# First routing of a retention + MoE + GLU kernel: counts of 32 bins by one product per tile of tokens, the digit by a product with ones

## The reference, cut to what matters

```python
logits = x @ w_gate                       # 3072 x 8
order = np.argsort(-logits.flatten())
for idx in order:                         # best pair first
    tok, e = idx // E, idx % E
    if assigned[tok] >= 0 or counts[e] >= cap: continue
    assigned[tok] = e; counts[e] += 1
h = np.maximum(x[mask] @ w1[e], 0.0); out[mask] = h @ w2[e]      # for each expert
y = (1 / (1 + np.exp(-(out @ w_gate2)))) * (out @ w_val) @ w_out
```

## Time and profile before

| | |
|---|---|
| median of 3 runs | 1074.85 us (1074.79 to 1075.24) |
| profiled execution, its own time | 1075.28 us |
| its span | 1073.5 us |
| PE busy | 1029.4 us (96%) |
| DVE busy | 704.0 us (66%) |
| ACT busy | 326.2 us (30%) |
| POOL busy | 122.6 us (11%) |
| moved by DMA | 107.69 MB |

### The profile page before, as it was taken

The page is one execution under the profiler, slowest core; times in us unless marked ns, Lnnn a source line. Parts: engine busy times, 40 slices in busy tenths (PEclk is TensorE's granted clock), DMA queues, the critical chain, the costliest instruction groups (busy, mean ns, idle before and its releaser), DMA issues.

```text
span 1073.5 us, 20171 instructions
## 1 busy us (share of the span) xinstructions
PE 1029.4 (96%) x7186; PEld 960.5 (89%) x7186; DVE 704.0 (66%) x1880; ACT 326.2 (30%) x622; POOL 122.6 (11%) x149
## 2 busy tenths in 40 slices
PE   8999728999999999999999999999999999999995
PEld 7888618989999999999999999999999999999995
DVE  4777778788678657765776577667765677554211
ACT  3222144412342234223332333223322341334110
POOL 4323301045200110010101010001001100110001
PEclk9999958999999999999999999999999999999998
DMA  9989765304230414132413232233214231423000
GB/s 204 211 211 224 170 201 155 111 4 140 77 116 21 128 55 134 39 89 79 131 58 89 79 119 70 61 106 109 80 48 120 89 99 40 128 70 117 2 1 29
DMA packets 197356, 107.69 MB, mean 100 GB/s; under 512 B 81936, under 2 KB 182800, under 8 KB 197264
## 3 DMA queue, kind: packets, MB, share of 16 engines
q1 hardware_dynamic: 193424, 93.94, 31.6%
q0 software_dynamic: 3840, 12.59, 3.7%
HBM read 88.41 MB, written 18.09 MB: 99 GB/s over the span
## 4 chain that ended last, share of the span: by engine, by line
PE 95%; DVE 3%; issue 1%; DMA 1%; POOL 0%; DVEq 0%; ACT 0%; POOLq 0%
PE bank L1382 21%; PE bank L1384 21%; PE bank L1383 21%; PE bank L1475 6%; PE bank L1476 6%; PE bank L1474 6%; PE bank L660 2%; PE bank L730 2%; PE bank L726 2%; PE bank L686 1%; PE bank L1329 1%; PE bank L693 1%; PE bank L740 1%; PE bank L638 1%; PE bank L707 1%
## 5 line engine op out<-in xcount | busy, mean ns | idle before, releaser
L1382 PE MATMUL bank<-h2h,resident 128*128 128x384 f32 x768 | 261.2, 340 | 0.0
L1384 PE MATMUL bank<-h2h,resident 128*128 128x384 f32 x768 | 257.9, 336 | 0.0
L1383 PE MATMUL bank<-h2l,resident 128*128 128x384 f32 x768 | 257.3, 335 | 0.0
L1382 PEld LDWEIGHTS bank<-h2h,resident 128*128 128x128 f32 x768 | 144.3, 188 | 2.9
L1383 PEld LDWEIGHTS bank<-h2l,resident 128*128 128x128 f32 x768 | 144.3, 188 | 2.9
L1384 PEld LDWEIGHTS bank<-h2h,resident 128*128 128x128 f32 x768 | 144.1, 188 | 0.0
L885 ACT ACTIVATE ring<-ring_raw 128x512 fp32r<-128x512 f32 x192 | 117.7, 623 | 54.7 <-DMA ring_raw<-in_moe_w_out_dram 43.1
L1202 DVE TENSOR_TENSOR pf<-bank,gate 128x384 f32<-128x384 f32 x96 | 53.5, 557 | 116.0 <-PE bank L1384 108.1
L1211 DVE TENSOR_TENSOR ring<-ring_raw,ring 128x512 fp32r<-128x512 f32 x192 | 128.7, 696 | 0.0
L909 ACT ACTIVATE ph<-pf 128x384 fp32r<-128x384 f32 x96 | 50.4, 525 | 257.5 <-DVE pf L1202 257.5
L1206 DVE TENSOR_TENSOR pl<-pf,ph 128x384 fp32r<-128x384 f32 x96 | 55.4, 577 | 56.8 <-ACT ph L909 56.8
(11 more groups left out here) (195 smaller groups left out, 1660.2 us busy)
## 6 DMA issues: line engine op xcount, KB each, us to landing
ring_raw<-in_moe_w_dram SPq DMA_DIRECT2D x128, 256.0 KB, 3.1
ring_raw<-in_moe_w_out_dram SPq DMA_DIRECT2D x64, 256.0 KB, 2.9
qraw<-in_q_dram SPq DMA_DIRECT2D x24, 256.0 KB, 4.1
kraw<-in_k_dram SPq DMA_DIRECT2D x24, 256.0 KB, 4.3
vraw<-in_v_dram SPq DMA_DIRECT2D x24, 256.0 KB, 4.4
xrows<-xrow SPq DMA_DIRECT2D x96, 64.0 KB, 2.1
xlaid<-xg SPq DMA_DIRECT2D x7, 768.0 KB, 4.5
zg<-xlaid SPq DMA_DIRECT2D x28, 192.0 KB, 4.2
```

The costliest lines, as they stand in the source:

```text
L1382: nc.tensor.matmul(ps, wh, xhi, start=start, stop=False)
L1383: nc.tensor.matmul(ps, wh, xlo, start=False, stop=False)
L1384: return nc.tensor.matmul(ps, wl, xhi, start=False, stop=stop)
```

## The change

In the first routing the products are taken one tile at a time: 24 products per digit, weights 32 columns (each fourth element of a group of `above_first`), moving columns the 8 of this tile, sums on 32 partitions of `PS_R`. The DVE reads these sums directly. `flag_first`, 32 flags in bf16, is multiplied with `ones` (32 rows, 128 columns), which gives the number of flags on all 128 partitions in one column of PSUM; `prefix` reads it there, and the tie step first copies it to `digit_at`. The copy to `partial`, the four products with `fold`, the table `fold` and the transposing reduction go. `FIRST_CHAIN` and `TABLES` are counts of the linked instructions and of the table instructions.

```diff
-        FIRST_CHAIN = 79
+        FIRST_CHAIN = 66
-        TABLES = 8 + 5 + 3 + 3
+        TABLES = 8 + 7 + 2
-        partial = sb("partial", [P, E, FOLD], F16)
+        flag_first = sb("flag_first", [P, 1], BF16)
-        fold = sb("fold", [P, FOLD, FOLD, RADIX], F16)
-                    fill(fold[:, :, :, :], 0.0)
-                    link(pool.affine_select(out=fold[:, :, :, :], in_=fold[:, :, :, :], compare_op=ALU.not_equal, fill=1.0,
-                                            base=0, pattern=[[-1, FOLD], [0, FOLD], [-FOLD, RADIX]], channel_multiplier=1))
             def first_threshold(j):
-                nc.vector.tensor_copy(partial[:, :, :], PS_R[:, 0:FOLD * E].rearrange("p (e t) -> p e t", e=E)).then_inc(partial_ready, 1)
-                dve.wait_ge(folded, j + 1)
-                link(nc.vector.tensor_tensor(reached[:, :], PS_K[:, 0:E], room[:, :], ALU.is_ge))
-                link(nc.vector.reduce_max(flag[:, :], reached[:, :], AX_X))
-                link(nc.vector.tensor_reduce(digit_at[:, :], flag[:, :].to_broadcast([P, RADIX]), axis=AX_X, op=ALU.add,
-                                             apply_transpose=True))
+                bins = slice(0, RADIX)
+                link(nc.vector.tensor_tensor(reached[bins, :], PS_R[bins, 0:E], room[bins, :], ALU.is_ge))
+                nc.vector.reduce_max(flag_first[bins, :], reached[bins, :], AX_X).then_inc(flagged, 1)
+                dve.wait_ge(flags_added, j + 1)
...
-                    link(nc.vector.scalar_tensor_tensor(prefix[:, :], digit_at[:, :].to_broadcast([P, U]), -float(RADIX),
+                    digit = PS_K[:, 0:1] if isinstance(i, int) and i == 0 else digit_at[:, :]
+                    link(nc.vector.scalar_tensor_tensor(prefix[:, :], digit.to_broadcast([P, U]), -float(RADIX),
                                                         raised[:, :], ALU.mult, ALU.add))
...
                 elif vis == V_TIE:
+                    if isinstance(i, int) and i == 0:
+                        link(nc.vector.tensor_copy(digit_at[:, :], PS_K[:, 0:1]))
...
-                    for t in range(0, U, FOLD):
+                    first = isinstance(i, int) and i == 0
+                    each = 1 if first else FOLD
+                    for t in range(0, U, each):
                         if t == 0:
                             pe.wait_ge(half_compared, i * DIGITS + vis + 1)
                         if t == U // 2:
                             pe.wait_ge(route_ready, i * (VISITS - 1) + vis + 1)
-                        if isinstance(i, int) and i == 0:
-                            bins = above_first[:, t // FOLD, :, :].rearrange("p r t -> p (r t)")
+                        if first:
+                            last = nc.tensor.matmul(PS_R[0:RADIX, 0:E], above_first[:, t // FOLD, :, t % FOLD], choice[:, :, t],
+                                                    start=t == 0, stop=t == U - 1)
...
-                    if isinstance(i, int) and i == 0:
-                        pe.wait_ge(partial_ready, vis + 1)
-                        for t in range(FOLD):
-                            last = nc.tensor.matmul(PS_K[:, 0:E], fold[:, t, :, :].rearrange("p k r -> p (k r)"), partial[:, :, t],
-                                                    start=t == 0, stop=t == FOLD - 1)
-                        last.then_inc(folded, 1)
+                    if first:
+                        pe.wait_ge(flagged, vis + 1)
+                        nc.tensor.matmul(PS_K[:, 0:1], ones[0:RADIX, :], flag_first[0:RADIX, :], start=True, stop=True).then_inc(flags_added, 1)
```

More of the change, by code:

```diff
@@ L222, in retention_moe_glu_kernel @@
         route_ready = sem("route_ready")
-        partial_ready = sem("partial_ready")
-        folded = sem("folded")
+        flagged = sem("flagged")
+        flags_added = sem("flags_added")
         half_compared = sem("half_compared")
@@ L1324, in visit @@
                             pe.wait_ge(route_ready, i * (VISITS - 1) + vis + 1)
-                        if isinstance(i, int) and i == 0:
-                            bins = above_first[:, t // FOLD, :, :].rearrange("p r t -> p (r t)")
-                        else:
-                            bins = above[:, t:t + FOLD, :].rearrange("p t r -> p (t r)")
-                        last = nc.tensor.matmul(PS_R[:, 0:FOLD * E], bins, choice[:, :, t:t + FOLD], start=t == 0, stop=t == U - FOLD)
+                        if first:
+                            last = nc.tensor.matmul(PS_R[0:RADIX, 0:E], above_first[:, t // FOLD, :, t % FOLD], choice[:, :, t],
+                                                    start=t == 0, stop=t == U - 1)
+                        else:
+                            last = nc.tensor.matmul(PS_R[:, 0:FOLD * E], above[:, t:t + FOLD, :].rearrange("p t r -> p (t r)"),
+                                                    choice[:, :, t:t + FOLD], start=t == 0, stop=t == U - FOLD)
                     last.then_inc(route_done, 1)
-                    if isinstance(i, int) and i == 0:
-                        pe.wait_ge(partial_ready, vis + 1)
-                        for t in range(FOLD):
-                            last = nc.tensor.matmul(PS_K[:, 0:E], fold[:, t, :, :].rearrange("p k r -> p (k r)"), partial[:, :, t],
-                                                    start=t == 0, stop=t == FOLD - 1)
-                        last.then_inc(folded, 1)
+                    if first:
+                        pe.wait_ge(flagged, vis + 1)
+                        nc.tensor.matmul(PS_K[:, 0:1], ones[0:RADIX, :], flag_first[0:RADIX, :], start=True, stop=True).then_inc(flags_added, 1)
                     return
```

## The result

The changed kernel takes 1077.87 us (median of 15 runs, 1076.71 to 1080.53) against 1075.10 (15 runs, 1074.28 to 1075.52): ratio 1.0027, interval 1.0021 to 1.0034. 1073.0 was forecast, with 0.09 for slower. The profiled execution took 1079.02, 1.15 above its kernel's median, so the differences read from its trace add up to more than the 2.77 between the medians; its span is 1077.0 against 1073.5.

A forecast was written before the change was run, and what follows sets the result against it. Routing's PE-DVE loop is all on the path, within a kernel mostly of untouched PE-bound rounds: 2.17 gained over seven digits, less 0.09 and 0.21, saves 1.87 from 1074.85, giving 1073.0 us; own range 1072.3 to 1073.7, 8-in-10 range 1071.8 to 1074.8.

The forecast's parts named there:

- Tables, buffers, shift: Setup and all behind the routing: dropping POOL's memset and select of fold changes nothing; clock shift at most 0.1 us lost.
- The slower case I named: Count products' strided weight loads at 54 ns each: digit 2.74 us, 2.7 us lost, 1077.5 us; chance 0.09.
- Behind the routing all is relative but the clock: After the first routing everything shifts earlier with it; only the clock's rise at about 169.0 us might stay fixed.
- The time around the span: Execution time outside the profiled span, taken as 1.78 us around 1073.50.
- The doubtful term: Weight loads of the 24 count products, elements 8 bytes apart: 27 ns from load to load, bounds 20 and 54.
- break-even of 38: Weight-load distance in ns in the count products at which the change would neither gain nor lose.
- the loop is all on the path: First routing's digit loop, 2.40 us a digit: every ns counts, only raised (some 0.2 us) is hidden.
- the hand-over by the ones product: From flag's end to prefix in each digit, one product with ones: 0.26 us, bounds 0.22 and 0.36.
- the split in halves: First twelve count products run on the compare's first half until 0.95 us, second half ready at 0.85: no stall.
- PSUM as prefix's source: Prefix reads its digit from PSUM instead of SBUF: nothing added, bounds -0.02 and 0.05 us.
- a change of form between products: PE switching between 128*32 and 32*128 forms: no gap expected; a refill at 0.1 us a digit would give 1073.7.
- the warmer clock: Rival in the routing loop: busier PE brings 2.4 GHz, loads 20 ns apart, 1.1 us less, 1071.9 us; chance 0.12.

The follow-up runs named there:

- on the grid: Large SBUF tiles start on a multiple of 256 bytes; the changed kernel with 32 or 1056 unused bytes ahead of them measured 1075.12 and 1075.39 us.
- The run in pairs: Changed kernel with 32 unused bytes, 13 extra DVE wait instructions and flags in pairs of tiles (weights 4 bytes apart): 1073.36 us, ratio 0.9984 against the kernel before.
- runs 4 and 1: Changed kernel with 32 unused bytes ahead of the large tiles (4): 1075.12 us; with 1056, restoring their old places (1): 1075.39 us.

## Why the prediction was wrong

**The step that failed** is "Tables, buffers, shift": "POOL's memset and select of fold go ... so nothing". I priced the removed buffers by the instructions that fill them and not by where everything behind them then lies. The runs put 2.35 to 2.75 us there: the change with its tiles on the grid is at 1075.12 and 1075.39, off it at 1077.87, and the old kernel moved off it is 2.35 slower. No rival had this mechanism. The slower case I named, weights at 54 ns and 1077.5, comes within 0.4 of the measured time by luck: its cause isn't there.

**"Behind the routing all is relative but the clock"** failed twice. Late data isn't relative: with slower loads POOL's splits ran into the preparation (+1.73). And the code's place isn't: the loop's DVE instructions stand 13 nearer the start, and stalls of 0.2 and 0.3 us appeared in each round, with 0.5 to 0.65 us lost over the rounds. Where they stood before, if anywhere, no trace shows.

**The time around the span** was taken as fixed ("1.78 around it"). It is 0.28 more in every version of the changed kernel.

**The doubtful term** was mis-sized: 27 ns from load to load, measured 33, which is 0.16 a digit and 1.1 in seven. It was named as doubtful and stayed under the break-even of 38, so it cost over half of the gain and not its sign. The rule weighed there, in the Trainium skill, "SBUF — State Buffer", "Specifications (TRN2)", that two hits in a 16-byte line give full bandwidth, isn't borne out for these weight loads: a load takes 116 ns with two hits and 103 with four, and 103 side by side too.

**What was right**: the loop is all on the path; the hand-over by the ones product 0.27 (0.26 forecast, where its own 0.28 and 0.167 give 0.25); the split in halves costs no stall; PSUM as prefix's source costs nothing (0.18); a change of form between products none. The seven digits and the copy brought 0.82; with the 1.1 of the loads they would have come to 1.9, the forecast's 1.87. The run in pairs has just that: its seven digits take 149.58 - 134.88 = 14.70 against 16.58, and its median is 1.92 below that of the kernel before. The terms also close on the grid: 1.87, less 1.1 for the loads, 0.5 to 0.65 for the stall and 0.28 around the span, is 0 to -0.2, and runs 4 and 1 measured 0.2 saved and 0.1 lost. The clock stayed at 0.50 in the loop, so the warmer clock fell too.

What stays open: why the DVE stalls at a place that depends on the number of instructions ahead. That the stalls go with the count is shown by two counts of inserted ones; that it is the supply of instructions is the likeliest reading and was not measured by itself. Open too are the 0.28 us around the span and the slow gathers.

## What to carry to other kernels

A removed or resized buffer moves all that is allocated behind it: compute the new byte offsets of the DMA's targets before and after an edit, and put them back where they were, here on multiples of 256, with an explicit pad. Compare two versions only when these offsets agree, otherwise a true gain of 0.1% drowns in a 0.25% artefact. When a gain shows at the start of a loop and not at its end, look in the waits for an engine that waits for itself, in a line that nobody touched. Compare the time outside the span too: a change can lose there what its trace shows as gained.

## What the runs showed of the hardware that I had not expected

DMA targets in SBUF off a multiple of 256 bytes: DMA share 1.07 at 222 GB/s where it was 0.96 at 227, and, in the changed kernel, 233 GB/s in the resident loads' stretch (136 to 150 us) where the same kernel on the grid has 304 and 309. Weight loads of 32 bf16 columns at half clock: 33 ns apart at a distance of 8 bytes, 27 at 4 bytes. A DVE loop body had stalls of 0.2 and 0.3 us that went when 7 or 13 instructions were put ahead of the loop. DVE instructions of 0.18 and 0.33 us took 1.12 and 0.93 beside POOL's splits of f32 tiles.
